# Low parts of a pair's second head a slot later, row maxima turned sooner and stored ahead of the deals, and the first head's maxima finished without the second head

## The reference

```
scores = scale * (q @ k.T)
thresh = max(scores, axis=-1) - tau            # tau = 0.02
scores = where(scores >= thresh, scores, -1e9)
attn   = exp(scores - max(scores)); attn = attn / (sum(attn) + 1e-9)
y      = attn @ v                              # then tokens x 512
x      = ((y @ w_a) * (y @ w_b)) @ w_out       # d_ff 1536
h = x @ w_in                                   # d_ff 1024
ln = layernorm(h * softmax(h)) * g
out = ln @ w_out2
```

## Time and profile before

| | |
|---|---|
| median of 3 runs | 1069.58 us (1069.33 to 1069.66) |
| the profiled execution | 1069.29 us, span 1067.1 us |
| TensorE busy in the span | 1001.3 us (94%), 5840 matmuls |
| DVE, ACT, POOL busy | 543.4, 415.1, 252.4 us |
| DMA, mean share of 16 engines | 24.9% of the span; 0.53 from 44.48 to 345.73 us |
| mean granted TensorE clock | 0.976 of full |

### The profile page before, as it was taken

One profiled execution on the slowest core, in us unless ns is written; L12 is line 12 of the kernel. 1 busy time (PEld: TensorE's weight loads), 2 busy tenths in 40 slices (PEclk: granted clock), 3 DMA queues, 4 the chain that ended last, 5 costly groups with the idle time before them and its releaser, 6 DMA issues.

```text
span 1067.1 us, 16652 instructions
## 1 busy us (share of the span) xinstructions
PE 1001.3 (94%) x5840; PEld 943.0 (88%) x5840; DVE 543.4 (51%) x862; ACT 415.1 (39%) x739; POOL 252.4 (24%) x242
## 2 busy tenths in 40 slices
PE   4899988999998889999999999999999999999998
PEld 4888878888887879999999999999999978888886
DVE  5676676677677675442122122222223485666564
ACT  2666656566665674431121121211212422322231
POOL 2666666566665670000000000000000000000000
PEclk8999998899999999999999999999999999999999
DMA  5545555454564425421001001000002200000000
GB/s 147 145 119 138 144 124 130 123 139 117 134 148 109 96 75 163 135 60 30 1 1 29 0 0 29 0 0 0 0 0 79 79 10 20 29 20 20 20 30 29
DMA packets 51578, 71.33 MB, mean 67 GB/s; under 512 B 14558, under 2 KB 24926, under 8 KB 51548
## 3 DMA queue, kind: packets, MB, share of 16 engines
q1 hardware_dynamic: 51548, 70.95, 24.9%
HBM read 33.25 MB, written 5.32 MB: 36 GB/s over the span
## 4 chain that ended last, share of the span: by engine, by line
PE 80%; issue 7%; DVE 4%; ACT 3%; DMA 2%; SPq 2%; POOL 2%; DVEq 0%; ACTq 0%; POOLq 0%
PE PS L1111 9%; PE PS L1112 9%; PE PS L1113 9%; PE PS L1094 8%; PE PS L1057 7%; PE PS L1059 5%; PE PS L1177 5%; PE PS L1176 5%; PE PS L1178 5%; PE PS L1235 3%; PE PS L1237 3%; PE PS L1236 3%; PE PS L1211 3%; PE PS L1209 3%; PE PS L1210 3%
## 5 line engine op out<-in xcount | busy, mean ns | idle before, releaser
L523 POOL TENSOR_TENSOR p_lo<-prob,p_hi 128x576 fp32r<-128x576 f32 x144 | 207.3, 1440 | 131.8 <-ACT p_hi L602 131.5
L1057 PE MATMUL PS<-ops 128*128 128x288 f32 x640 | 192.6, 320 | 47.7 <-DVE neg_max L820 29.2
L1111 PE MATMUL PS<-x_hi,w_ab_rolled 128*128 128x384 f32 x576 | 192.5, 334 | 1.4 <-issue 1.4
L1112 PE MATMUL PS<-x_lo,w_ab_rolled 128*128 128x384 f32 x576 | 192.4, 334 | 0.0
L1113 PE MATMUL PS<-x_hi,w_ab_rolled 128*128 128x384 f32 x576 | 192.4, 334 | 0.0
L1059 PE MATMUL PS<-ops 128*128 128x288 f32 x640 | 185.2, 308 | 0.0
L1057 PEld LDWEIGHTS PS<-ops 128*128 128x128 f32 x640 | 129.2, 202 | 61.4 <-DVE neg_max L820 36.4
L931 DVE TENSOR_TENSOR gate<-gate,PS 128x384 f32<-128x384 f32 x72 | 39.9, 554 | 253.0 <-ACT gate L701 253.0
L820 DVE TENSOR_REDUCE neg_max<-PS 128x1 f32<-128x576 f32 x144 | 108.6, 756 | 92.8 <-PE PS L1059 91.6
L701 ACT ACTIVATE gate<-PS 128x384 f32<-128x384 f32 x72 | 35.4, 491 | 268.2 <-PE PS L1113 268.2
L1059 PEld LDWEIGHTS PS<-ops 128*128 128x128 f32 x640 | 129.5, 202 | 0.0
(11 more groups left out here) (89 smaller groups left out, 1546.8 us busy)
## 6 DMA issues: line engine op xcount, KB each, us to landing
qk_raw<-qkT_dram SPq DMA_DIRECT2D x32, 288.0 KB, 2.8
ops<-qk_hi SPq DMA_DIRECT2D x62, 144.0 KB
ops<-qk_hi SPq DMA_DIRECT2D x31, 288.0 KB
ops<-qk_lo SPq DMA_DIRECT2D x62, 144.0 KB
v_raw<-v_tiles_dram SPq DMA_DIRECT2D x32, 160.0 KB, 2.4
xT<-head_sb SPq DMA_DIRECT2D x32, 144.0 KB, 2.4
out_dram<-o_sb SPq DMA_DIRECT2D x18, 256.0 KB, 2.0
stage<-inverse_dram SPq DMA_DIRECT2D x20, 192.0 KB, 3.8
```

What stands on the lines that cost most here:

```text
L523: pool.tensor_tensor(p_lo[:, r, :], prob[:, s % RAW, :], p_hi[:, r, :].bitcast(F32), ALU.subtract).then_inc(p_lo_done, 1)
L1057: pe.matmul(ps[:, b, 0:HALF], weights[0][:, r, own], moving[0][:, r, cols], start=(n == 0), stop=False)
L1111: pe.matmul(bank, w[:, 0, :], x_hi[:, k, :], start=(k == 0), stop=False)
L1112: pe.matmul(bank, w[:, 0, :], x_lo[:, k, :], start=False, stop=False)
```

## The change

Seven edits. (1) DVE makes the low parts of a second head in slot 7 instead of 6, and inverts the sums in slot 6 instead of 7. (2) DVE turns the maxima of the next pair's first head in slot 4, behind the mask, instead of slot 5; those of its second head in slot 8, behind the mask, instead of slot 0 of the next step, ahead of the mask. (3) SP stores the maxima ahead of each of the two deals of a step, and loads them right behind the deal. (4) SP stores the inverse ahead of the load of q and k. (5) The deals of heads 1 to 3 leave out the zeros, which POOL's first memset has written, and `dealt` counts one DMA less for them. (6) At the start the load of head 2 stands ahead of the deal of head 1, that of head 3 right behind it, the store of head 0's maxima ahead of head 2's low parts. (7) Head 0's part of its fifth score tile is made once more by itself, right after tile 3, in the third PSUM buffer (four matmuls and one reduction more), so that head 0's maxima are complete before head 1's operands are there; head 0's and head 1's maxima are turned sooner.

```diff
--- before.py
+++ after.py
@@ -187,6 +187,8 @@
         v_hi_set = sem("v_hi_set")
         v_lo_set = sem("v_lo_set")
         s_done = sem("s_done")
+        short_done = sem("short_done")
+        short_max = sem("short_max")
         max_done = sem("max_done")
         max_hi_done = sem("max_hi_done")
         max_split = sem("max_split")
@@ -295,7 +297,8 @@
 
         def dealt(i, j):
 
-            return DEALT * (i + j // ROLL + (1 if j % ROLL else 0))
+
+            return DEALT * (i + j // ROLL) + (DEALT - 16 if j % ROLL else 0)
 
         max_dram = nc.dram_tensor("max_dram", (heads, LANES, P), F32, kind="Internal").ap()
         inverse_dram = nc.dram_tensor("inverse_dram", (heads // PAIR, P, PAIR * S // P), F32, kind="Internal").ap()
@@ -342,7 +345,8 @@
 
 
                 at_least(sp, st_done, number(i - 1, j // 2, MID + 1 if j % 2 == 0 else SLOTS))
-                deal_zeros(i, j)
+                if not (isinstance(i, int) and i == 0):
+                    deal_zeros(i, j)
                 deal_high(i, j)
                 deal_low(i, j)
 
@@ -397,8 +401,8 @@
 
             def step(i, e):
 
+                head(store_max, i, e, 1)
                 head(deal, i, e + 1, 1)
-                head(store_max, i, e, 1)
                 head(load_max, i, e, 1)
                 head(load_qk, i, e + 3, 0)
                 head(load_v, i, e + 1, 0)
@@ -406,12 +410,12 @@
                 head(move_head, i, e - 1, 1)
                 pair(spread_sums, i, e - 1)
 
+                head(store_max, i, e + 1, 0)
                 head(deal, i, e + 2, 0)
-                head(store_max, i, e + 1, 0)
+                head(load_max, i, e + 1, 0)
                 head(load_v, i, e + 1, 1)
-                head(load_max, i, e + 1, 0)
+                pair(store_inverse, i, e - 1)
                 head(load_qk, i, e + 3, 1)
-                pair(store_inverse, i, e - 1)
                 head(move_head, i, e, 0)
 
             load_qk(0, 0)
@@ -420,19 +424,20 @@
             sp.dma_start(tau_in[:, :], tau.to_broadcast([P, 1])).then_inc(consts_in, 16)
             sp.dma_start(gain[:, :], g_col).then_inc(consts_in, 16)
             sp.wait_ge(consts_set, CONSTS)
-            deal_zeros(0, 1)
+            sp.wait_ge(first_ops, FIRST_OPS)
+            load_qk(0, 2)
             deal_high(0, 1, qk_hi_done)
             deal_low(0, 1)
-            load_qk(0, 2)
+            load_qk(0, 3)
             load_v(0, 0)
-            deal_zeros(0, 2)
             deal_high(0, 2, qk_hi_done)
-            load_qk(0, 3)
+            store_max(0, 0)
             deal_low(0, 2)
+
+            sp.wait_ge(s_done, NT)
+            load_max(0, 0)
             load_v(0, 1)
-            store_max(0, 0)
             load_qk(1, 0)
-            load_max(0, 0)
             load_qk(1, 1)
             for i in range(2):
                 for e in range(2):
@@ -674,7 +679,9 @@
             act.wait_ge(first_ops, FIRST_OPS)
             high_qk(0, 2)
             act.wait_ge(consts_set, CONSTS + 3)
-            high_max(0, 0)
+
+            act.wait_ge(short_max, 1)
+            act.activation(max_cols[:, 0:NT], neg_max[:, 0, 0:NT], ACT.Copy).then_inc(max_hi_done, 1)
             high_qk(0, 3)
             high_max(0, 1)
 
@@ -864,20 +871,20 @@
                     if exists(ei, ee):
                         score_max(ei, ee, es)
                     ni, ne = pair_at(i, e + 1)
-                    if s == 0:
-                        turn_max(i, 2 * e + 1)
-                    if s == 5 and exists(ni, ne):
-                        turn_max(ni, 2 * ne)
                     if s > 0:
                         mask(i, e, s - 1)
                     elif not (isinstance(i, int) and 2 * i + e == 0):
                         mask(*pair_at(i, e - 1), SLOTS - 1)
+                    if s == MID and exists(ni, ne):
+                        turn_max(ni, 2 * ne)
+                    if s == SLOTS - 1 and exists(ni, ne):
+                        turn_max(ni, 2 * ne + 1)
                     mi, me = pair_at(i, e + 2)
                     if s == 2 and exists(mi, me):
                         low_qk(mi, 2 * me)
-                    if s == 6 and exists(mi, me):
+                    if s == 7 and exists(mi, me):
                         low_qk(mi, 2 * me + 1)
-                    if s == 7 and not (isinstance(i, int) and 2 * i + e == 0):
+                    if s == 6 and not (isinstance(i, int) and 2 * i + e == 0):
                         invert(*pair_at(i, e - 1))
                     if isinstance(i, int) and (2 * i + e, s) == (PAIRS - 2, SLOTS - 1):
 
@@ -898,10 +905,15 @@
             dve.wait_ge(ones_set, 4)
             for s in range(MID):
                 score_max(0, 0, s, first_ps[s % 3])
+
+            dve.wait_ge(short_done, 1)
+            dve.tensor_reduce(out=neg_max[:, 0, MID:NT], in_=first_ps[2][:, :, 0:HALF], axis=AX_XY, op=ALU.max,
+                              negate=True).then_inc(short_max, 1)
             low_qk(0, 2)
+            turn_max(0, 0)
+
             score_max(0, 0, MID, first_ps[MID % 3])
             score_max(0, 0, MID + 1, first_ps[(MID + 1) % 3])
-            turn_max(0, 0)
             for s in range(MID + 2, SLOTS):
                 score_max(0, 0, s, first_ps[s % 3])
             score_max(0, 1, 0, first_ps[SLOTS % 3])
@@ -909,6 +921,7 @@
             dve.tensor_scalar(neg_tau[:, :], tau_in[:, :], -1.0 / SCALE, None, ALU.mult).then_inc(tau_ready, 1)
             dve.wait_ge(tau_ready, 1)
             low_qk(0, 3)
+            turn_max(0, 1)
             last = heads // ROLL - 1
             for i in range(2):
                 for e in range(2):
@@ -1046,10 +1059,10 @@
 
         @block.tensor
         def _(pe):
-            def product(ps, e, s, weights, moving, done):
-
-
-                parts = operands(e, s)
+            def product(ps, e, s, weights, moving, done, heads_in=PAIR):
+
+
+                parts = operands(e, s)[:heads_in]
                 for b in range(2):
                     for n, (r, tile, whole) in enumerate(parts):
                         own = slice(tile, tile + P)
@@ -1142,7 +1155,12 @@
             pe.wait_ge(qk_lo_done, 1)
             for s in range(SLOTS):
                 at_least(pe, max_done, s - 2)
+                if s == MID + 1:
+                    pe.wait_ge(short_max, 1)
                 scores(0, 0, s, first_ps[s % 3])
+                if s == MID - 1:
+                    pe.wait_ge(max_done, 3)
+                    product(first_ps[2], 0, MID, (qq, qx), (kk, kx), short_done, 1)
             pe.wait_ge(max_done, SLOTS - 2)
             scores(0, 1, 0, first_ps[SLOTS % 3])
             last = heads // ROLL - 1
```

## The result

The changed kernel takes 1072.43 us (median of 9 runs, 1070.69 to 1075.28) against 1069.66 us (9 runs, 1067.97 to 1070.25) for the kernel before: ratio 1.0027, 95% interval 1.0017 to 1.0037. It is slower by 0.27%, where 1066.3 us was forecast and "faster" had the largest chance, 0.45. The profiled execution is the fastest of the nine: 1070.69 us, span 1068.4 us.

A forecast was written before the change was run, and what follows sets the result against it. TensorE, busy 94% of the span, bounds the kernel, so only its waits and lower-clock time can be won; 3.8 - 5.9 - 1.4 - 1.8 + 2.0 = -3.3 us gives 1066.3 us, own range 1062.5 to 1070.

The forecast's parts named there:

- Low parts in slot 7: DVE's slot 7: TensorE's 1.91 us wait for the reduction goes, while the low parts still collide with POOL.
- What is late next: the deal: Slot 8: the first head's deal, issued 2.15 us later behind the store of the maxima, becomes TensorE's wait, +0.27 us.
- rival B: In the loop the wait really goes, as deals need less than 6.6 us: 1031 us or less; chance 0.06.
- U to R: From the start of slot 3's scores to TensorE's restart in slot 8: +0.27 us a pair, +3.8 for 14 pairs.
- R to U: From TensorE's restart in slot 8 to the start of slot 3's scores: -0.45 us for each of 13 pairs, -5.9.
- The second deal: Slot 3's scores wait for it behind store and transpose, starting 10.0 to 10.1 us after slot 8's restart: -5.9 us.
- rival A: Two waits a pair, the clock falling after both, or milder, slower deals: slower, together put at 1072 us; chance 0.20.
- The small wait: Before the second head's first product with v: TensorE's 0.68 us wait for ACT's copy goes, -0.84 us.
- The start: Kernel start: head 2's q and k load sooner, winning about half of a 3.12 us wait, -1.4 us.
- The last deal: Last pairs: the last second-head deal goes out sooner as the inverse is stored a slot earlier, -1.8 us.
- The last transpose: Step of pair 14: DVE transposes the last maxima ahead of normalize, delaying the mask TensorE awaits, +2.0 us.
- a third of 13: Milder slowing: deals taking 7.16 us in most pairs give +13 us, 1079 at worst, 1072 for a third of it.

## Why the prediction was wrong, point by point

*Low parts in slot 7.* Right: no wait of TensorE names DVE's reduction in the loop any more, and the low parts still meet POOL (1.28 us at 227.80, beside 1.42 of POOL from 227.04; 0.76 alone).

*What is late next: the deal.* Right. The restart in the loop waits for the DMA of `ops` (predicted 2.2 us, measured 2.0 to 2.7). Putting the stores behind the deals gives 37 us, the gain that rival B, at 0.06, had for the change as it is. B's reason, that a deal is faster when the queue ahead of it is emptier, is not what it takes: there too the first deal is used 6.72 us after its issue (220.54 to 227.26) and the second 6.75 (230.10 to the next U at 236.85), only the first is issued 2.4 us sooner. For the same reason the forecast's thought that the store also holds up the deal's bytes finds no support: two neighbouring first deals of the loop are used 6.66 and 6.75 us after their issue with a store ahead, and 6.72 and 6.57 without. What each edit would do without the other was not asked in the forecast; it should have been.

*Two terms failed, by about the same amount.* By the stretches of the two profiled executions:

| term | before | after | predicted | measured |
|---|---|---|---|---|
| U to R, 14 times, mean | 12.70 | 13.23 | +3.8 | +7.5 |
| R to U, 13 times, mean | 10.47 | 10.30 | -5.9 | -2.3 |
| start, to the U before the first R | 31.84 | 29.72 | -1.4 | -2.1 |
| last R to its U | 13.29 | 10.97 | -1.8 | -2.3 |
| that U to the wait for the mask | 17.06 | 17.67 | +2.0 | +0.6 |
| sum | | | -3.3 | +1.4 |

*The +3.8 us of U to R* was 0.27 us a pair for 14, and was 0.54. In the first steps, which are written out, the forecast holds: 12.92 (52.69 to 65.61), as predicted, and 12.88 to 13.12 in all six that are written out for SP. In SP's loop, the other eight, it is 13.37 to 13.65. There the handovers from engine to engine are longer. DVE and SP in an early step, then in the loop:

```profile
57.92 0.22 DVE L835 STREAM_TRANSPOSE max_turn<-max_cols 128x32 f32<-128x32 f32 x1 [0.77 <-POOL max_cols L536]
58.16 0.64 SPq L356 DMA_DIRECT2D max_dram<-max_turn  x1
58.84 0.65 SPq L325 DMA_DIRECT2D ops<-zeros  x1
```

```profile
222.34 0.21 DVE L835 STREAM_TRANSPOSE max_turn<-max_cols 128x32 f32<-128x32 f32 x1 [1.03 <-POOL max_cols L536]
...
222.72 0.66 SPq L356 DMA_DIRECT2D max_dram<-max_turn  x1
...
223.54 0.66 SPq L325 DMA_DIRECT2D ops<-zeros  x1
```

From the start of the transpose to the deal it is 0.92 us in the one and 1.20 in the other, where the prediction had 0.96. It allowed 0.06 or 0.05 for a handover, not read from a row of the loop; the rows show 0.02 and 0.04 (transpose to store, store to deal) in the early step and 0.17 and 0.16 in the loop. The transpose itself starts 5.23 us after U (52.69) in the one and 5.52 (216.82) in the other, where 5.34 was forecast, and the deal is used 6.77 and 6.66 after its issue: 12.92 and 13.38 in all. In the chain of waits of a loop step a register instruction stands between the two DMAs:

```profile
209.28 0.66 SPq L356
...
209.98 0.07 SPq L33
210.10 0.66 SPq L325
```

In the loop the value waited for is worked out in registers, which is the likely reason; no run here tests it. It is not so at every handover: in the kernel before, the deal that waits for TensorE alone goes out 4.28 us after U in the first written-out step (54.01 to 58.29) and 4.14 after it in the loop (217.23 to 221.37).

*The second deal, -5.9 us*, was -0.45 a pair, and was -0.17. In the five pairs with the clock at 1.00 R to U has a mean of 10.11 us, as the 10.0 to 10.1 of the forecast, with the wait of 1.70 in slot 3 (predicted 1.6). In the eight where the clock has fallen it is 10.42. There the forecast saw no wait, for TensorE's own work, put at 10.1, would fill the time. That work is 9.8 us (the run with only the first store ahead), and there is a wait, 0.71 at 240.76: the matmuls from the restart on are already slow, so that the reduction and the mask move, and with them the transpose (2.77 us after R at 230.20, 2.20 after R at 206.69) and the deal (3.92 after R, for 3.41). That is rival A's way of slowing, though not by a second fall of the clock, which rose as a whole.

*A reading.* The forecast's 10.75 us for R to U ends at 240.63, which is the second matmul of slot 3; U is at 240.50, and the stretch is 10.62.

*The small wait* went, as forecast. *The start* gave 0.7 us more than predicted in the profiled execution; by itself it gave 1.2 to 2.5. *The last deal* gave 0.5 more. *The last transpose* cost 1.4 less, since normalize runs faster with less of POOL beside it. All three misses were to the good.

The sum was a small difference of terms of 4 to 6 us, and errors of 0.3 us in two stretches that come 14 and 13 times turned its sign. The median, 1072.43, lies outside the 1062.5 to 1070 that the forecast gave as its own range, and inside the 1061.5 to 1073 of all rivals together. Rival A, at 0.20, had 1072, but that agreement is luck: the clock in the loop rose from 0.94 to 0.96 instead of falling, no deal of the loop took 7.16 us, and A's own "a third of 13" on 1066.3 is 1070.6 and not 1072.

## What to carry to other kernels

A queue that issues DMAs in order is an engine like the others: what stands ahead of a critical DMA with a wait of its own delays it by that wait, even if it moves only 16 KB. When a wait is removed, look at what was hidden behind it, and then ask of each part of the change whether it helps or hurts that next thing; here one part of two lines was worth 30 us and another took them back. A term that comes once a pair wants its handovers read from rows of the loop itself, and its size taken as a mean over all pairs.

## What the runs showed of the hardware

From DVE's transpose over a store to the next DMA it took 0.28 us more in the loop than in the steps written out (1.20 against 0.92); the loop's awaited values are in registers, and that this is the reason is not tested. A deal of 884 KB in six DMAs took 6.75 us from its first issue to its use, and 6.31 with 147 KB less. TensorE's work from R to U took 8.29 us with the clock at 1.00 and 9.81 with its mean at 0.83. A wait of 3.99 us in TensorE was followed by a stretch at clock 0.78, and taking it away won 6.4 us, of which the wait itself is the greater part. Four operations of DVE took 4.40 us with three of POOL beside them and 3.19 with one.
